# Attention on one Trainium2 core: the value products cut in three parts, one in each slot of the loop

## The chip, the core and the metric

The kernel runs on one core of one Trainium2 chip. TensorE (PE) multiplies, VectorE (DVE) and ScalarE (ACT) empty PSUM and do the element work, GpSimd (POOL) prepares operands and issues some DMAs, SyncE (SP) issues the rest. PSUM has eight banks of 128 x 512 fp32. The metric is the device time of one execution in microseconds (us).

## The reference, cut to what matters

The program is an attention block (16 heads of 768 x 64, scores masked by a hash of queries and keys), then a Fourier mixing layer with an MLP, then a second mixing layer. The change touches the attention alone:

```
q_bits = (einsum('bhsd,dk->bhsk', q, proj) > 0);  k_bits likewise
mask   = q_bucket[:, :, :, None] == k_bucket[:, :, None, :]
scores = where(mask, q @ k.T / sqrt(64), -1e9)
attn   = exp(scores - max);  attn /= sum(attn) + 1e-9
out    = attn @ v
```

## The kernel before, in words

**Slots.** Each head has six tiles of 128 query rows against 768 keys. schedule() makes a list of slots, one for each tile n = 6h + t, and every engine walks that list in order. "Slot t of head h" below is the slot of tile n. In it stand, for each engine:

- PE: four score products of tile n (L765, L766, into one of two pairs of banks), six transposes of the exponentials of tile n - 2 (L740, two ring banks named eta and etb), then value products if the slot has any (L779, L780), then its units: "bits" (three hash products of a half of the next head's queries and keys, L718 to L720 with 24 columns) or "back" (three transposes of a finished half of the output, L751).
- DVE: the row maximum (L984) and the affine pair of tile n (L987), the low halves ETL of tile n - 2 (L994), and for a back unit the inverse sums and the addition OS (L1014 to L1020).
- ACT: the high halves ETH of tile n - 2 (L613), the exponential of tile n (L633), copies for units (MB L622, OL L627), and OS, the copy of finished value products out of PSUM (L642).

fp32 data are split in a high part that the multiplier takes whole and the rest: ETH and ETL, TOPH and TOPL, VHL (both parts of v side by side).

**Value products.** A head has two of them, (h, 0) and (h, 1), one for each half of its query rows: 12 matmuls of 384 columns into one ring bank. Before the change (h, 0) stands whole in slot 5 of head h, and (h, 1) whole in slot 2 of head h + 1. The last matmul raises s_pv.

**The ring.** The eta, etb, bits, back and value products take the four banks 4 to 7 in turn; take_bank() waits until the engine that empties the bank four units ago has done so.

**GpSimd's queue.** It runs in program order, once per head: split_top(h + 1), which writes TOPH and TOPL of the next head (L498, L500); mask_rows, MR (L505); finish(h - 1, 0), which scales an output half into X (L513); split_v(h + 1), VHL (L529, L531), which waits until s_pv shows that all value products of head h - 1 are done, since it overwrites their VHL; scale_q(h + 2) on QK (L490); finish(h - 1, 1). In the first eight heads a table or weight DMA is issued twice a head (L556). The bits products of a head wait for its TOPH and TOPL (s_top), and its score products for the mask rows and for DMAs that SP issues once TOPL and the bits are there.

Of the kernel before, what the change touches and what calls it, by code (L numbers as in the profile page):

```python
# [7 lines left out]
ACT = mybir.ActivationFunctionType  # L8
# [5 lines left out]
NH = B * H  # L14
# [20 lines left out]
FOLD = [NH * QT + 2 + i for i in range(3)]  # L35
LAG = 2
NE = LAG + 1
RING = 4
NSTAT = 4 * QT
TG = 5  # L40
WIDTHS = (P, P, 1, P, P - 1)
# [8 lines left out]
def schedule():  # L50


    slots = [(None, None, None, [("bits", 0, i) for i in range(2)])]
    for n in range(NH * QT + 5):
        h, t = divmod(n, QT)
        pv = (h - 1, 1) if t == 2 and h else (h, 0) if t == 5 and h < NH else None
        units = []
        if h + 1 < NH and t == 1:
            units += [("bits", h + 1, i) for i in range(2)]
        if h and t in (1, 4):  # L60
            units.append(("back", h - 1, t // 4))
        slots.append((n if n < NH * QT else None, n - LAG if LAG <= n < NH * QT + LAG else None, pv, units))
    return slots


def program(nc, qk, v, projb, w1, w2, wth, wtr, wti, wch, ident_in, gamma_in, sign_in, cs_in, ss_in, alt_in, cd_in, sd_in, out):
# [126 lines left out]
    with ctx:  # L193
# [11 lines left out]
            return PS[:, 4 + u % RING, :]  # L205


        def blocks(ap):
            return ap.rearrange("p (a b) -> p a b", b=P)

# [2 lines left out]
        for _, et, pv, us in slots:  # L213
            if et is not None:
                units += [("eta", *divmod(et, QT)), ("etb", *divmod(et, QT))]
            if pv is not None:
                units.append(("pv", *pv))
            units += us
        unit_no = {u: i for i, u in enumerate(units)}
        done = {}  # L220
        for u in units:
            done[u] = len([w for w in done if w[0] != "pv"]) + 1
        nth, seen = {}, {}
        for u in units:
            seen[u[0]] = nth[u] = seen.get(u[0], 0) + 1
# [247 lines left out]
        def _(pool):  # L473
# [18 lines left out]
            def split_top(h):  # L492
                b = h % 2
                pool.wait_ge(s_sq, h)
                pool.wait_ge(s_top, 2 * h)
                if h >= 2:
                    pool.wait_ge(s_s, QT * (h - 1))
                nc.gpsimd.tensor_copy(TOPH[:, b], QK[:, b]).then_inc(s_top, 1)  # L498
                pool.wait_ge(s_top, 2 * h + 1)
                nc.gpsimd.tensor_tensor(TOPL[:, b], QK[:, b], TOPH[:, b].bitcast(F32), ALU.subtract).then_inc(s_top, 1)  # L500

            def mask_rows(h):
                pool.wait_ge(emptied["bits"], 2 * (h + 1))
                pool.wait_ge(s_mask, 32 * h)
                nc.gpsimd.tensor_scalar(MR[:], MB[:], gamma[:, 0:1], gamma[:, 1:2], ALU.is_gt, ALU.mult).then_inc(s_mr, 1)  # L505
# [29 lines left out]
            scale_q(1)  # L535
            for slot, (tile, et, pv, us) in enumerate(slots):
                h, t = divmod(slot - 1, QT)
                if slot and t == 0 and h + 1 < NH:
                    split_top(h + 1)
                if slot and t == 1:  # L540
                    if h + 1 < NH:
                        mask_rows(h + 1)
                    if h:
                        finish(h - 1, 0)
                if slot and t == 2:
                    if h == 0:
                        split_v(0)
                    if h + 1 < NH:
                        split_v(h + 1)
                    if h + 2 < NH:  # L550
                        scale_q(h + 2)
                if slot and t == 4 and h:
                    finish(h - 1, 1)
                if slot and t in (3, 5) and early:
                    dst, src, landed = early.pop(0)
                    pool.dma_start(dst, src).then_inc(landed, 16)  # L556
            pool.wait_ge(s_pv, 2 * NH)
            split_low(n_w1)
            for n in range(NT):
# [27 lines left out]
        def _(act):  # L587
# [16 lines left out]
            for slot, (tile, et, pv, us) in enumerate(slots):  # L604
                if et is not None:
                    h, t = divmod(et, QT)
                    for k, kind in enumerate(("eta", "etb")):
                        u = unit_no[kind, h, t]
                        bank = blocks(ring(u)[:, 0:HC])
                        act.wait_ge(s_ring, done[kind, h, t])  # L610
                        if h and k == 0:
                            act.wait_ge(s_pv, 2 * h + t // HALF - 1)
                        nc.scalar.activation(ETH[:, t // HALF, k * HALF:(k + 1) * HALF, (t % HALF) * P:(t % HALF + 1) * P],  # L613
                                             bank, ACT.Copy).then_inc(s_eth, 1)
                for u in us:
                    kind, h, i = u
                    c = slice(i * HC, (i + 1) * HC)
                    if kind == "bits" and h:
                        act.wait_ge(s_ring, done[u])
                        if h >= 2:  # L620
                            act.wait_ge(s_mr, h - 1)
                        nc.scalar.activation(MB[:, c], ring(unit_no[u])[0:2 * NM, 0:HC], ACT.Copy).then_inc(emptied["bits"], 1)  # L622
                    elif kind == "back":
                        act.wait_ge(s_ring, done[u])
                        if h:
                            act.wait_ge(emptied["back"], nth[u] - 2)
                        nc.scalar.activation(OL2[:, i], blocks(ring(unit_no[u])[:, 0:HC])[:, :, D:P], ACT.Copy).then_inc(s_ol, 1)  # L627
                if tile is not None:
                    t = tile % NSTAT
                    act.wait_ge(s_sb, tile + 1)  # L630
                    if tile >= NE:
                        act.wait_ge(s_ring, done["etb", (tile - NE) // QT, (tile - NE) % QT])
                    nc.scalar.activation(E[:, tile % NE, :], s_bank(tile)[:, 0:S], ACT.Exp, bias=affine[:, t, 1:2],  # L633
                                         scale=affine[:, t, 0:1], accum_out=esum[:, t:t + 1]).then_inc(s_exp, 1)
                if slot in FOLD[1:]:
                    fold_high(0, FOLD.index(slot) - 1)
                if pv is not None:
                    h, c = pv
                    act.wait_ge(s_pv, 2 * h + c + 1)
                    if h >= 1:  # L640
                        act.wait_ge(s_ring, done["back", h - 1, c])
                    nc.scalar.activation(OS[:, c, :], ring(unit_no["pv", h, c])[:, 0:HC], ACT.Copy).then_inc(emptied["pv"], 1)  # L642

            for b in range(B):
                for g in range(TG):
# [69 lines left out]
        def _(pe):  # L715
# [38 lines left out]
            for tile, et, pv, us in slots:  # L754
                if tile is not None:
                    h, t = divmod(tile, QT)
                    pe.wait_ge(s_away, 32 * (h + 1))
                    pe.wait_ge(s_in, 32 * (h + 1))
                    pe.wait_ge(s_mask, 32 * (h + 1))
                    if tile >= 2:  # L760
                        pe.wait_ge(s_exp, tile - 1)
                    c = slice(t * P, (t + 1) * P)
                    for lo, hi in ((0, 512), (512, S)):
                        dst = s_bank(tile)[:, lo:hi]
                        nc.tensor.matmul(dst, TOPL[:, h % 2, c], TOPH[:, h % 2, lo:hi], start=True, stop=False)  # L765
                        last = nc.tensor.matmul(dst, QM[:, h % 2, c], KM[:, h % 2, lo:hi], start=False, stop=True)  # L766
                    last.then_inc(s_s, 1)
                if et is not None:
                    unit(("eta", *divmod(et, QT)))
                    unit(("etb", *divmod(et, QT)))  # L770
                if pv is not None:
                    h, c = pv
                    pe.wait_ge(s_vs, 2 * h + 2)
                    pe.wait_ge(emptied["eta"], h * QT + (c + 1) * HALF)
                    pe.wait_ge(emptied["etb"], h * QT + (c + 1) * HALF)
                    take_bank(unit_no["pv", h, c])
                    bank = ring(unit_no["pv", h, c])
                    for j in range(QT):
                        nc.tensor.matmul(bank[:, 0:HC], VHL[:, h % 2, j, :], ETH[:, c, j, :], start=(j == 0), stop=False)  # L779
                        last = nc.tensor.matmul(bank[:, 0:HC], VHL[:, h % 2, j, :], ETL[:, c, j, :], start=False, stop=(j == QT - 1))  # L780
                    last.then_inc(s_pv, 1)
                for u in us:
                    unit(u)

# [11 lines left out]
            for b in range(B):  # L796
# [18 lines left out]
                if b:  # L815
                    norm_transpose(0)
                    norm_transpose(1)
                else:
                    pe.wait_ge(emptied["back"], seen["back"])

                def cosines(dst, cols):
                    for g in range(2):
# [414 lines left out]
```

## Time and profile before

| | us |
|---|---|
| median of 3 runs | 825.1 (821.96 to 827.07) |
| the profiled execution | 824.21, span 821.4 |
| attention, first score product to last ETL | 14.2 to 279.3 of the span |
| PE busy / DVE / ACT / POOL in the span | 753.2 / 451.6 / 313.2 / 269.5 |

The times in the rows are from the start of the span. A row of the timeline gives the start, the duration, engine, line, operation, output and inputs, shapes, and the number of instructions merged in it; in brackets stands how long the engine had been idle before it and what ended that. A matmul's duration holds its way through the array, so the pitch, from one start to the next, is what it occupies.

### The profile page before, as it was taken

The numbers are of one execution on the slowest core, as the hardware profiler recorded it, in microseconds if no ns is written. First come the engines' busy times: TensorE is split into PE (matmuls) and PEld (weight loads), VectorE is DVE, ScalarE is ACT, GpSimd is POOL, SyncE is SP. The second block draws the span as 40 slices with busy tenths as digits, with TensorE's granted clock in tenths as the row PEclk, the third lists the DMA queues.
The fourth block names the chain that finished last, engine by engine and source line by source line (L and its number), as shares of the span: only waits on it lengthen the run. The fifth ranks groups of instructions, "written<-read, shape, count | busy, mean of one in ns | idle before, by whom it ended". The sixth has DMA issues, their size and how long they took to land.

```text
span 821.4 us, 11002 instructions
## 1 busy us (share of the span) xinstructions
PE 753.2 (92%) x3826; PEld 624.3 (76%) x3826; DVE 451.6 (55%) x834; ACT 313.2 (38%) x659; POOL 269.5 (33%) x243
## 2 busy tenths in 40 slices
PE   4899899999999679699999999999996898999998
PEld 2778787878788556588888888888884787888876
DVE  2888889888888967722222111211117665756433
ACT  2787877788778602210110111111113433222201
POOL 3867677656662167453200000110001214221100
PEclk9999999999999966889999999999999999999999
DMA  5354546543321023631100000400003222000002
GB/s 147 96 144 114 149 110 186 173 105 98 84 72 43 1 102 129 204 103 40 39 1 0 1 1 0 129 14 1 0 1 90 78 58 71 1 14 13 26 26 77
DMA packets 44680, 56.26 MB, mean 68 GB/s; under 512 B 15956, under 2 KB 27860, under 8 KB 44116
## 3 DMA queue, kind: packets, MB, share of 16 engines
q1 hardware_dynamic: 38100, 41.65, 18.3%
q0 software_dynamic: 6528, 13.92, 5.8%
q8 instruction: 32, 0.52, 0.3%
q14 instruction: 20, 0.16, 0.1%
HBM read 38.65 MB, written 3.15 MB: 51 GB/s over the span
## 4 chain that ended last, share of the span: by engine, by line
PE 75%; DVE 19%; issue 3%; DMA 1%; ACT 1%; SPq 1%; POOL 0%; ACTq 0%; POOLq 0%
PE PS L718 19%; PE PS L720 18%; PE PS L719 18%; DVE negmax L984 6%; DVE ETL L994 5%; PE PS L779 4%; PE PS L780 3%; PE PS L765 3%; DVE affine L987 3%; PE PS L740 3%; PE PS L766 3%; PE PS L898 1%; PE PS L751 1%; PE PS L905 1%; PE PS L790 1%
## 5 line engine op out<-in xcount | busy, mean ns | idle before, releaser
L1109 DVE SCALAR_TENSOR_TENSOR HL<-PS,HH 128x512 fp32r<-128x512 f32 x48 | 33.2, 692 | 189.2 <-ACT HH L681 189.2
L633 ACT ACTIVATE E<-PS,affine 128x768 f32<-128x768 f32 x96 | 95.6, 995 | 42.0 <-DVE affine L987 42.0
L984 DVE TENSOR_REDUCE negmax<-PS 128x1 f32<-128x768 f32 x96 | 91.2, 951 | 34.8 <-PE PS L766 34.7
L681 ACT ACTIVATE HH<-PS 128x512 fp32r<-128x512 f32 x48 | 28.7, 598 | 210.5 <-PE PS L720 210.5
L994 DVE TENSOR_TENSOR ETL<-PS,ETH 128x384 fp32r<-128x384 f32 x192 | 97.1, 547 | 1.0 <-ACT ETH L613 1.0
L613 ACT ACTIVATE ETH<-PS 128x384 fp32r<-128x384 f32 x192 | 83.2, 489 | 10.8 <-PE PS L740 10.5
L740 PE MATMUL PS<-ident,E 128*128 128x128 f32 x576 | 81.7, 274 | 0.0
L765 PE MATMUL PS<-TOPH,TOPL 128*128 128x512 f32 x192 | 71.4, 372 | 10.3 <-DMA KM<-MR 6.0
L718 PE MATMUL PS<-UTH,W1H 128*128 128x512 f32 x192 | 76.7, 400 | 2.1 <-DVE UTL L1092 2.1
L720 PE MATMUL PS<-UTH,W1L 128*128 128x512 f32 x192 | 75.8, 395 | 0.0
L719 PE MATMUL PS<-UTL,W1H 128*128 128x512 f32 x192 | 75.7, 394 | 0.0
L720 PE MATMUL PS<-W2H,HL 128*128 128x512 f32 x192 | 74.7, 389 | 0.0
L718 PE MATMUL PS<-W2H,HH 128*128 128x512 f32 x192 | 74.7, 389 | 0.0
L719 PE MATMUL PS<-W2L,HH 128*128 128x512 f32 x192 | 74.7, 389 | 0.0
L779 PE MATMUL PS<-ETH,VHL 128*128 128x384 f32 x192 | 67.3, 350 | 3.5 <-DVE ETL L994 1.7
L740 PEld LDWEIGHTS PS<-ident,E 128*128 128x128 f32 x576 | 65.6, 141 | 3.4 <-DVE ETL L994 3.4
L581 POOL TENSOR_TENSOR ZF<-X,SC 128x512 f32<-128x512 f32 x24 | 30.5, 1291 | 106.9 <-ACT SC L702 106.9
L780 PE MATMUL PS<-ETL,VHL 128*128 128x384 f32 x192 | 64.8, 338 | 0.0
L766 PE MATMUL PS<-KM,QM 76*128 76x512 f32 x192 | 62.6, 346 | 0.0
L505 POOL TENSOR_SCALAR MR<-MB,gamma 24x768 fp32r<-24x768 f32 x15 | 44.1, 2942 | 51.0 <-ACT MB L622 51.0
L718 PE MATMUL PS<-ZH,WTH 128*128 128x512 f32 x144 | 59.8, 415 | 0.0
L720 PE MATMUL PS<-ZH,WTL 128*128 128x512 f32 x144 | 57.0, 396 | 0.0
(167 smaller groups left out, 1516.8 us busy)
## 6 DMA issues: line engine op xcount, KB each, us to landing
stage<-in_moe_w_ch_dram SPq DMA_DIRECT2D x36, 256.0 KB, 2.6
QK<-in_qk_dram SPq DMA_DIRECT2D x16, 384.0 KB, 3.8
W1H<-in_moe_w_ch_dram POOLq DMA_DIRECT2D x4, 1024.0 KB, 5.7
W2H<-in_moe_w_ch_dram POOLq DMA_DIRECT2D x4, 1024.0 KB, 8.8
QM<-TOPH SPq DMA_DIRECT2D x16, 192.0 KB, 2.8
KM<-TOPL SPq DMA_DIRECT2D x16, 192.0 KB, 3.1
TOPL<-QM SPq DMA_DIRECT2D x16, 192.0 KB, 2.7
TOPH<-TOPH SPq DMA_DIRECT2D x16, 192.0 KB, 3.0
```

The lines of the kernel that those rows point to most:

```text
L613: nc.scalar.activation(ETH[:, t // HALF, k * HALF:(k + 1) * HALF, (t % HALF) * P:(t % HALF + 1) * P], bank, ACT.Copy).then_inc(s_eth, 1)
L633: nc.scalar.activation(E[:, tile % NE, :], s_bank(tile)[:, 0:S], ACT.Exp, bias=affine[:, t, 1:2], scale=affine[:, t, 0:1], accum_out=esum[ ...
L718: nc.tensor.matmul(dst, hl, hr, start=start, stop=False)
L719: nc.tensor.matmul(dst, hl, lr, start=False, stop=False)
L720: return nc.tensor.matmul(dst, ll, hr, start=False, stop=stop)
L740: last = nc.tensor.transpose(bank[:, j * P:(j + 1) * P], E[:, tile % NE, (first + j) * P:(first + j + 1) * P], ident[:])
L765: nc.tensor.matmul(dst, TOPL[:, h % 2, c], TOPH[:, h % 2, lo:hi], start=True, stop=False)
L766: last = nc.tensor.matmul(dst, QM[:, h % 2, c], KM[:, h % 2, lo:hi], start=False, stop=True)
L779: nc.tensor.matmul(bank[:, 0:HC], VHL[:, h % 2, j, :], ETH[:, c, j, :], start=(j == 0), stop=False)
L780: last = nc.tensor.matmul(bank[:, 0:HC], VHL[:, h % 2, j, :], ETL[:, c, j, :], start=False, stop=(j == QT - 1))
L984: nc.vector.tensor_reduce(negmax[:, t, 1:2], s_bank(tile)[:, 0:S], AX_X, ALU.max, negate=True).then_inc(s_max, 1)
L994: nc.vector.tensor_tensor(ETL[where], blocks(ring(unit_no[kind, h, t])[:, 0:HC]), ETH[where].bitcast(F32), ALU.subtract).then_inc(emptied[ ...
```

## The change

The value products of a half are cut in three parts of four matmuls. With PVLAG = 5 the part of tile p = n - 5 stands in slot n, so every slot from the fifth on has one: parts 2 and 3 of (h - 1, 0) in slots 0 and 1 of head h, those of (h - 1, 1) in slots 2, 3 and 4, and part 1 of (h, 0) in slot 5. All of them accumulate in a bank of their own, OT (bank 7), and the first part of a half waits until ACT has copied the half before out of it. The ring has three banks, without the value products. Units are one a slot at most: bits in slots 0 and 1 (both were in slot 1), back in slots 3 and 5 (they were in 1 and 4). On ACT the exponential now stands ahead of the copies OS, MB and OL. On GpSimd, split_top(h + 2) stands in slot 5 of head h where split_top(h + 1) stood in slot 0, and the finish calls come later.

```diff
-RING = 4
+RING = 3
+PVLAG = 5
...
-    for n in range(NH * QT + 5):
+    for n in range(NH * QT + QT):
         h, t = divmod(n, QT)
-        pv = (h - 1, 1) if t == 2 and h else (h, 0) if t == 5 and h < NH else None
         units = []
-        if h + 1 < NH and t == 1:
-            units += [("bits", h + 1, i) for i in range(2)]
-        if h and t in (1, 4):
-            units.append(("back", h - 1, t // 4))
+        if h + 1 < NH and t < 2:
+            units.append(("bits", h + 1, t))
+        if h and t in (3, 5):
+            units.append(("back", h - 1, t // 5))
+        p = n - PVLAG
+        pv = (p // QT, p % QT // HALF, p % HALF) if 0 <= p < NH * QT else None
...
+        OT = PS[:, 7, 0:HC]
...
-                if slot and t == 0 and h + 1 < NH:
-                    split_top(h + 1)
-                if slot and t == 1:
-                    if h + 1 < NH:
-                        mask_rows(h + 1)
-                    if h:
-                        finish(h - 1, 0)
+                if slot and t == 0:
+                    if h == 0:
+                        split_top(1)
+                    elif h > 1:
+                        finish(h - 2, 1)
+                if slot and t == 1 and h + 1 < NH:
+                    mask_rows(h + 1)
                 if slot and t == 2:
...
                         split_v(h + 1)
                     if h + 2 < NH:
                         scale_q(h + 2)
-                if slot and t == 4 and h:
-                    finish(h - 1, 1)
-                if slot and t in (3, 5) and early:
+                if slot and t == 3 and h:
+                    finish(h - 1, 0)
+                if slot and t == 5 and h + 2 < NH:
+                    split_top(h + 2)
+                if slot and t in (2, 4) and early:
...
+            finish(NH - 1, 1)
...
-                if pv is not None:
-                    h, c = pv
-                    act.wait_ge(s_pv, 2 * h + c + 1)
-                    if h >= 1:
-                        act.wait_ge(s_ring, done["back", h - 1, c])
-                    nc.scalar.activation(OS[:, c, :], ring(unit_no["pv", h, c])[:, 0:HC], ACT.Copy).then_inc(emptied["pv"], 1)
+                if pv is not None and pv[2] == HALF - 1:
+                    h, c, _ = pv
+                    act.wait_ge(s_pv, 2 * h + c + 1)
+                    if h:
+                        act.wait_ge(s_ring, done["back", h - 1, c])
+                    nc.scalar.activation(OS[:, c, :], OT, ACT.Copy).then_inc(emptied["pv"], 1)
...
-                    h, c = pv
-                    pe.wait_ge(s_vs, 2 * h + 2)
-                    pe.wait_ge(emptied["eta"], h * QT + (c + 1) * HALF)
-                    pe.wait_ge(emptied["etb"], h * QT + (c + 1) * HALF)
-                    take_bank(unit_no["pv", h, c])
-                    bank = ring(unit_no["pv", h, c])
-                    for j in range(QT):
+                    h, c, part = pv
+                    if part == 0:
+                        pe.wait_ge(s_vs, 2 * h + 2)
+                        pe.wait_ge(emptied["eta"], h * QT + (c + 1) * HALF)
+                        pe.wait_ge(emptied["etb"], h * QT + (c + 1) * HALF)
+                        if h or c:
+                            pe.wait_ge(emptied["pv"], 2 * h + c)
+                    for j in range(2 * part, 2 * part + 2):
...
-                    last.then_inc(s_pv, 1)
+                    if part == HALF - 1:
+                        last.then_inc(s_pv, 1)
```

GpSimd's queue before, with the semaphores that each instruction waits for (s_pv: value products done; s_sum: back additions done; s_qk0: queries and keys loaded). The piece begins in slot 1 of a head, at the mask rows:

```order
L505 TENSOR_SCALAR MR<-MB,gamma 24x768 [waits s_mask,s_bits]
L513 TENSOR_TENSOR X<-OS_68,einv 128x3x64 [waits s_sum,s_inv]
L529 CAST VHL<-VR 128x6x64 [waits s_pv,s_v1]
L531 TENSOR_TENSOR VHL<-VR,VHL 128x6x64 [waits s_vs]
L490 TENSOR_SCALAR QK<-QK 64x768 [waits s_qk0]
L556 DMA W1H<-in_moe_w_ch_dram 128x2048
L513 TENSOR_TENSOR X<-OS_68,einv 128x3x64 [waits s_sum,s_inv]
L556 DMA W1H<-in_moe_w_ch_dram 128x2048
L498 CAST TOPH<-QK 128x768 [waits s_s,s_top,s_sq]
L500 TENSOR_TENSOR TOPL<-QK,TOPH 128x768 [waits s_top]
```

The same stretch now, from the mask rows of the same head (line numbers shift by two to six):

```order
L507 TENSOR_SCALAR MR<-MB,gamma 24x768 [waits s_mask,s_bits]
L531 CAST VHL<-VR 128x6x64 [waits s_pv,s_v1]
L533 TENSOR_TENSOR VHL<-VR,VHL 128x6x64 [waits s_vs]
L492 TENSOR_SCALAR QK<-QK 64x768 [waits s_qk0]
L560 DMA W1H<-in_moe_w_ch_dram 128x2048
L515 TENSOR_TENSOR X<-OS_68,einv 128x3x64 [waits s_sum,s_inv]
L560 DMA W1H<-in_moe_w_ch_dram 128x2048
L500 CAST TOPH<-QK 128x768 [waits s_s,s_top,s_sq]
L502 TENSOR_TENSOR TOPL<-QK,TOPH 128x768 [waits s_top]
L515 TENSOR_TENSOR X<-OS_68,einv 128x3x64 [waits s_sum,s_inv]
```

From VHL to TOPL the instructions are the same but for their finish: one X stood before VHL and one between the DMAs; now one stands between the DMAs and one behind TOPL.

PE now, from the end of slot 5 of one head to the first bits product in slot 0 of the next; the value products of slot 5 wait for s_os, the copy of the half before out of OT, and the bits product for s_top:

```order
L785 MATMUL PS<-ETH,VHL 128x384 [waits s_etb,s_os,s_eta,s_vs]
L786 MATMUL PS<-ETL,VHL 128x384
L785 MATMUL PS<-ETH,VHL 128x384
L786 MATMUL PS<-ETL,VHL 128x384
L756 MATMUL PS<-ident,OS 128x128 [waits s_os,s_etb]
L756 MATMUL PS<-ident,OS 128x128 x2
L770 MATMUL PS<-TOPH,TOPL 128x512 [waits s_mask,s_exp,s_in,s_away]
...
L785 MATMUL PS<-ETH,VHL 128x384
L786 MATMUL PS<-ETL,VHL 128x384
L723 MATMUL PS<-TOPH,projH 24x384 [waits s_top,s_sum]
```

Before, slot 5 had twelve value products in one row and slot 0 none, and the bits stood one slot later, behind the transposes of slot 1.

## Rows read from the trace of the kernel before

**Rows 1.** Busy time in a stretch: us, PE, PEld, DVE, ACT, POOL, clock, DMA
```profile
140.00:180.00 40.00, 36.86 (x229) 31.46 (x228) 35.62 (x75) 31.18 (x72) 25.99 (x23) 1.00 0.46 132
```

**Rows 2.** Timeline of PE, slots 1 to 4 of head 7
```profile
134.59 0.55 PE L751 MATMUL PS<-ident,OS 128*128 128x128 f32 x3 [0.61 <-DVE ETL L994]
134.89 0.48 PE L765 MATMUL PS<-TOPH,TOPL 128*128 128x512 f32 x1
...
136.25 0.42 PE L779 MATMUL PS<-ETH,VHL 128*128 128x384 f32 x1
136.51 0.34 PE L780 MATMUL PS<-ETL,VHL 128*128 128x384 f32 x1
...
138.43 0.39 PE L765 MATMUL PS<-TOPH,TOPL 128*128 128x512 f32 x1
...
139.13 0.82 PE L740 MATMUL PS<-ident,E 128*128 128x128 f32 x6
139.71 0.48 PE L765 MATMUL PS<-TOPH,TOPL 128*128 128x512 f32 x1
```

**Rows 3.** Timeline of DVE, the same head
```profile
132.92 0.95 DVE L984 TENSOR_REDUCE negmax<-PS 128x1 f32<-128x768 f32 x1
134.91 0.16 DVE L1014 TENSOR_SCALAR einv<-esum 128x3 f32<-128x3 f32 x1
135.88 0.96 DVE L984 TENSOR_REDUCE negmax<-PS 128x1 f32<-128x768 f32 x1
140.32 0.81 DVE L987 SCALAR_TENSOR_TENSOR affine<-negmax 128x2 f32<-128x2 f32 x1
```

**Rows 4.** Timeline of POOL, the same head
```profile
138.73 0.50 POOL L529 CAST VHL<-VR 128x384 fp32r<-128x384 f32 x1 [0.45 <-PE PS L780]
140.29 2.13 POOL L490 TENSOR_SCALAR QK<-QK 64x768 f32<-64x768 f32 x1
144.75 0.50 POOL L513 TENSOR_TENSOR X<-OS,einv 128x192 f32<-128x192 f32 x1 [1.75 <-DVE OS L1020]
145.21 0.60 POOL L556 DMA_DIRECT2D W1H<-in_moe_w_ch_dram  x1
145.81 0.84 POOL L498 CAST TOPH<-QK 128x768 fp32r<-128x768 f32 x1
146.74 1.83 POOL L500 TENSOR_TENSOR TOPL<-QK,TOPH 128x768 fp32r<-128x768 f32 x1
```

**Rows 5.** Timeline of ACT, the same head
```profile
137.11 1.01 ACT L633 ACTIVATE E<-PS,affine 128x768 f32<-128x768 f32 x1
138.63 0.49 ACT L642 ACTIVATE OS<-PS 128x384 f32<-128x384 f32 x1 [0.42 <-PE PS L780]
```

**Rows 6.** The DMAs on POOL, by tile: ns min/median/max; two of ten rows
```profile
L556 POOL DMA_DIRECT2D W1H<-in_moe_w_ch_dram x4: 594/604/618, 125.8 to 145.2; - x4
L556 POOL DMA_DIRECT2D CSH<-in_cs_dram x1: 874/874/874, 42.2 to 42.2; - x1
```

**Rows 7.** Timeline: first bits products of heads 2 and 15, TOPL of head 2, last ETL
```profile
29.95 1.83 POOL L500 TENSOR_TENSOR TOPL<-QK,TOPH 128x768 fp32r<-128x768 f32 x1
32.51 0.42 PE L718 MATMUL PS<-TOPH,projH 128*24 128x384 f32 x1
...
248.23 0.42 PE L718 MATMUL PS<-TOPH,projH 128*24 128x384 f32 x1
...
277.38 1.95 DVE L994 TENSOR_TENSOR ETL<-PS,ETH 128x384 fp32r<-128x384 f32 x4 [1.01 <-ACT ETH L613]
```

**Rows 8.** Timeline of PE, behind gaps; then a stretch of PE: busy, granted clock, DMA, GB/s
```profile
345.10 0.45 PE L790 MATMUL PS<-ident,UN 128*128 128x128 f32 x1 [3.29 <-DVE UTL L1092]
...
634.99 0.52 PE L905 MATMUL PS<-ident,nat 128*128 128x128 f32 x3 [1.73 <-DVE TR L1141]
...
688.57 0.52 PE L905 MATMUL PS<-ident,nat 128*128 128x128 f32 x3 [2.21 <-DVE WTL L1131]
...
344.50:354.60 10.10, 7.38 (x21) 0.50 0.46 131
689.30:692.50 3.20, 3.20 (x11) 0.50 0.09 31
```

More of the change, by code:

```diff
@@ L215, in program @@
                 units += [("eta", *divmod(et, QT)), ("etb", *divmod(et, QT))]
-            if pv is not None:
-                units.append(("pv", *pv))
             units += us
@@ L221, in program @@
         for u in units:
-            done[u] = len([w for w in done if w[0] != "pv"]) + 1
+            done[u] = len(done) + 1
         nth, seen = {}, {}
@@ L614, in _ @@
                                              bank, ACT.Copy).then_inc(s_eth, 1)
+                if tile is not None:
+                    t = tile % NSTAT
+                    act.wait_ge(s_sb, tile + 1)
+                    if tile >= NE:
+                        act.wait_ge(s_ring, done["etb", (tile - NE) // QT, (tile - NE) % QT])
+                    nc.scalar.activation(E[:, tile % NE, :], s_bank(tile)[:, 0:S], ACT.Exp, bias=affine[:, t, 1:2],
+                                         scale=affine[:, t, 0:1], accum_out=esum[:, t:t + 1]).then_inc(s_exp, 1)
+                if slot in FOLD[1:]:
+                    fold_high(0, FOLD.index(slot) - 1)
+                if pv is not None and pv[2] == HALF - 1:
[4 more added lines that the diff above has]
+                    nc.scalar.activation(OS[:, c, :], OT, ACT.Copy).then_inc(emptied["pv"], 1)
                 for u in us:
@@ L627, in _ @@
                         nc.scalar.activation(OL2[:, i], blocks(ring(unit_no[u])[:, 0:HC])[:, :, D:P], ACT.Copy).then_inc(s_ol, 1)
[L628 to L637, printed above, removed]
-                    h, c = pv
-                    act.wait_ge(s_pv, 2 * h + c + 1)
-                    if h >= 1:
-                        act.wait_ge(s_ring, done["back", h - 1, c])
-                    nc.scalar.activation(OS[:, c, :], ring(unit_no["pv", h, c])[:, 0:HC], ACT.Copy).then_inc(emptied["pv"], 1)
             for b in range(B):
@@ L771, in _ @@
                 if pv is not None:
-                    h, c = pv
-                    pe.wait_ge(s_vs, 2 * h + 2)
-                    pe.wait_ge(emptied["eta"], h * QT + (c + 1) * HALF)
-                    pe.wait_ge(emptied["etb"], h * QT + (c + 1) * HALF)
-                    take_bank(unit_no["pv", h, c])
-                    bank = ring(unit_no["pv", h, c])
-                    for j in range(QT):
-                        nc.tensor.matmul(bank[:, 0:HC], VHL[:, h % 2, j, :], ETH[:, c, j, :], start=(j == 0), stop=False)
-                        last = nc.tensor.matmul(bank[:, 0:HC], VHL[:, h % 2, j, :], ETL[:, c, j, :], start=False, stop=(j == QT - 1))
-                    last.then_inc(s_pv, 1)
+                    h, c, part = pv
[6 more added lines that the diff above has]
+                    for j in range(2 * part, 2 * part + 2):
+                        nc.tensor.matmul(OT, VHL[:, h % 2, j, :], ETH[:, c, j, :], start=(j == 0), stop=False)
+                        last = nc.tensor.matmul(OT, VHL[:, h % 2, j, :], ETL[:, c, j, :], start=False, stop=(j == QT - 1))
+                    if part == HALF - 1:
+                        last.then_inc(s_pv, 1)
                 for u in us:
@@ L819, in _ @@
                     pe.wait_ge(emptied["back"], seen["back"])
+                    pe.wait_ge(emptied["pv"], 2 * NH)
                 def cosines(dst, cols):
```

## The prediction, made before the changed kernel ran

> **What bounds it now.** I read three views: busy time by stretch, then the timelines of one head, engine by engine, then PE's idle times and its clock. In the middle of the attention PE is busy 36.9 of 40 us, DVE 35.6, ACT 31.2, at full clock [rows 1]. So no engine is alone the bound. The unit is the head: from the first bits product of head 2 (in head 1) to that of head 15 (in head 14) lie 248.23 - 32.51 = 215.7 us for 13 heads, 16.6 a head [rows 7].
>
> What must PE do in a head? From the pitches: score products 138.43 to 139.13, 0.70; six transposes 139.13 to 139.71, 0.58; twelve value products 136.25 to 138.43, 2.18, that is 0.26 for the first behind transposes and 0.175 for each other; a back unit 0.30 [rows 2], and the score product behind it is 0.08 dearer, as one behind transposes is. Bits matmuls have the same 384 columns: three are 0.52. What must DVE do? A slot without back is 132.92 to 134.91, 2.0; the back work 134.91 to 135.88 adds 1.0 [rows 3]. Before, PE has a slot of S + T + 2.18 = 3.5 us where DVE has only 2.0 to do, and slots where DVE needs longer than PE: neither can be busy all the time. That is what an even spread of the value products removes.
>
> **The change, first by engine loads alone.** PE's slots become 0.70 + 0.58 + 0.26 + 3 x 0.175 = 2.05 bare, 2.57 with bits, 2.43 with back: 2 x 2.57 + 2 x 2.05 + 2 x 2.43 = 14.1 a head. DVE's: 6 x 2.0 + 2 x 1.0 = 14.0, and about 1.1 more of affine instructions held up while GpSimd works: one is 0.81 long [rows 3], where the others are 0.16, and two or so a head are. So by loads a head could take 15.1 instead of 16.6.
>
> Does DVE's hold-up stay? The row shows an affine held 0.65 beside the QK scaling, which runs 2.13 [rows 3, 4]. The Trainium skill (SBUF — State Buffer, two separate sides) says that a VectorE instruction with two SBUF inputs and a GpSimd instruction exclude each other for the whole instruction; by that the row would be over 2 long, and the head 15.1 + 1.3 = 16.4, most of the gain gone. Here the affine came free 0.8 after the scaling began, so the row speaks for a part of it only, and I keep 1.1.
>
> **Then by waits: GpSimd's queue.** split_v(h + 1) stands in front of scale_q(h + 2), finish(h - 1, 0) and split_top(h + 2), and waits for the last value product of head h - 1. That stood in slot 2 of head h; VHL was written 0.30 after its end (138.43 to 138.73), having waited 0.45 [rows 2, 4]. Now its last part is in slot 4: two slots later. And the one who waits for split_top(h + 2), the bits product, has gone from slot 1 of the next head to slot 0, one slot earlier. Before, TOPL of head 2 was there at 31.78 and its bits came at 32.51 [rows 7]: 0.7 of slack in the whole head. The change takes about three slots from it. I follow the loop:
>
> - GpSimd, from the end of the value products in slot 4: 0.30 to VHL; VHL and the QK scaling, 138.73 to 142.42, 3.69; one finish 0.46 (144.75 to 145.21); TOPH and TOPL 145.81 to 148.57, 2.76; the signal to PE about 0.1. Sum 7.3 [rows 4].
> - PE, from that same point to where the bits are due: slot 5, 2.43, slot 0, 2.05, so 4.5; and 0.4 of wait for OT (below). PE stands idle 7.3 - 4.9 = 2.4 us at the bits.
> - PE, from the bits to the next end of slot 4: 0.52 + 2.57 + 2.05 + 2.43 + 2.05 = 9.6. DVE in slots 1 to 4 has 9.0, begins 1.2 behind the bits, and needs its backs at 3.0, so it keeps up with PE. The period is 9.6 + 7.3 = 16.9.
> - In heads 1 to 7 two DMAs stand in the chain, 0.59 to 0.87 each, a little under 0.04 of it beside other work [rows 6]: 14 of them, 9.3 in all, 1.3 a head, period 18.2. Before, they lay in GpSimd's slack.
>
> So 13 periods: 13 x 16.9 + 9.3 = 229.0 against 215.7: **+13.3**.
>
> The ends. Bits of head 1 now stand between the first two score tiles, at low clock (0.96); the mask rows and all behind them on GpSimd come about 1.15 later, and TOPL of head 2 at 32.9 instead of 31.78: **+0.5**. After the bits of head 15 nothing waits for GpSimd. Before, 248.23 to the end of the last ETL, 279.33, took 31.1 [rows 7]. Now: to the first score tile of head 15, 0.52 + 2.57 + 2.05 + 2.43 + 2.05 + 2.43 and 0.4 for OT, 12.4; five slots, by DVE 11.0; the last tile to its ETL 5.6 (score 0.7, DVE's queue 3.0 and twice 0.95). Sum 29.0: **-2.1**. Behind that the fold of the first batch sets the pace as before, and the last back now comes behind more ACT work; I cost it at 0, from -0.5 to +1.
>
> Costed at nothing, and by what: the ring of three. The second transposes of a slot need the bank that DVE empties a slot earlier, due 0.5 to 1.0 us before. ACT has 1.8 for ETH and E a slot and is not full [rows 1, 5]. The mask rows reach their DMAs about 8 us after the bits, and score products need them 12 after. If one of these covers fails it costs 0.3 to 0.8 a head.
>
> The wait for OT, for which no row exists: lower bound 0 (PE comes later than the copy), upper bound E and OS behind a late maximum. In slot 4 DVE starts its maximum 0.5 late, because the back add of slot 3 is before it; then 1.15 to the affine's end, E 1.0, OS 0.5 [rows 3, 5] makes it 0.4 later than PE arrives in slot 5. It falls in the shadow of the GpSimd chain, so its 0.4 only shortens the idle time above.
>
> Sum on the profiled execution's 824.2: 13.3 + 0.5 - 2.1 = +11.7, 835.9, if the clock stays.
>
> **The clock.** PE is now idle 2.4 us once a head, 3.7 with the DMAs. Gaps of 2.21 and 3.29 were followed by stretches at a granted clock of 0.50, that is 1.2 GHz, of 3 and 10 us; one of 1.73 was not [rows 8]. At half the clock a slot with bits grows by about 0.44 (bits) + 0.70 (score) + 0.55 (value) = 1.7, on 2.57; over some 3.4 us that is 1.3 to 1.6 lost, and it lies in the 9.6 of the loop, so it counts in full. I take it for 5 of the 7 long gaps and 3 of the 6 short ones (2.4 lies near the row of 2.21, and one row is no rule), 8 x 1.4, less a quarter that falls into the gap itself: **+8**. Bounds: 0, and 13 x 1.6 = 21. The Trainium skill (TensorE: Matmul & The Clock Gate, on oscillation) warns against idle gaps, and by its rule the short gaps are harmless and the DMA heads at the edge; that would give +0 to +9, and the row of 2.21 speaks against its harmless part.
>
> **Forecast:** 824.2 + 11.7 + 8 = 844; the profiled execution is 0.9 below the median of the runs, which is inside the rounding; I say 844. Attention ends near 299 instead of 279.
>
> **Rivals.**
> - *The chain is there, the clock holds*: 836 to 838. For it: the gap of 1.73, after which it held [rows 8]; against it, the other two. Chance 0.20; the forecast with some falls (839 to 849) 0.48.
> - *Falls in nearly every head*, by the 2.21 row: 824.2 + 11.7 + 16 to 21 = 852 to 857. Chance 0.14.
> - *Faster: the chain does not bind.* If TOPL is ready when PE comes to the bits, loads decide: 15.1 a head, 1.5 less for 14 heads, 824 - 21 = **804**. It decides at a chain under 4.9 us from the end of slot 4; the rows give 7.3. It would need s_pv to be satisfied earlier than the order of the queues says. Chance 0.05.
> - *Little change*: the loop is there, but the tail and the clock behind the attention fall well (the three runs differ by 5 us), and PE's slots are shorter than I add: 826 to 833. Chance 0.10. The remaining 0.03 is a loss from a cover gone (ring, mask DMAs): up to 865.
>
> About 1% is what one can tell here. Faster by over 1% (under 817): 0.05. Within: 0.10. Slower: 0.85. The range, 831 to 857, leaves out the fast case, most of the small change and the top.
>
> **What would show it.** GpSimd's VHL cast ended by PE's value product once a head, with an idle time of several us; PE's first bits product (24 columns) in slot 0 idle 2 to 4 us, ended by GpSimd's TOPL; heads 18 to 20 us apart up to head 7 and 17 to 18 after it; less busy DVE and PE in each head. DVE waiting for PE once a head. Heads 14 and 15 shorter than before. Wrong if the bits do not wait for TOPL, if the period is under 16.5, or if the clock falls and the period is unmoved by it.

## The result, and the profile after

The changed kernel takes 847.3 us (median of 4 runs, 844.1 to 856.6) against 824.3; the ratio is 1.030, 95% interval 1.021 to 1.038. Forecast were 844 and a range of 831 to 857. The profiled execution took 848.04, its span 845.3 instead of 821.4.

Where do the 23.9 us of the spans lie? The last ETL ends at 306.86; before, at 279.33 [rows 7]. So the attention is 27.5 longer, and all that follows 3.6 shorter, in which nothing was changed: its low-clock stretches fall differently from execution to execution, 44 us of them before and 38 now. I therefore compare attention ends from here on, and give the times beside them.

First the page of the changed kernel: busy time, then the chain that ended last.

```profile
PE 752.8 (89%) x3826; PEld 629.7 (74%) x3826; DVE 455.6 (54%) x834; ACT 318.4 (38%) x659; POOL 268.0 (32%) x243
...
PE 75%; POOL 12%; DVE 5%; issue 3%; ACT 2%; DMA 1%; SPq 1%; POOLq 0%; ACTq 0%
```

The same work as before, to 2%. But the chain goes through POOL for 12% of the span where it had 0%, and through DVE for 5% instead of 19%. Which waits are new? From the list of waits: engine, line and who ended them; us in total, times, longest.

```profile
POOL VHL L531 <- PE PS L786: 38.9, 14, 3.3
...
PE PS L723 <- POOL TOPL L502: 35.5, 14, 3.6
```

These two are the loop: GpSimd waits 14 times for the last value product (the VHL cast), then TensorE 14 times for TOPL. One turn of it, POOL's timeline in heads 11 and 12, which have no DMAs:

```profile
223.31 1.80 POOL L502 TENSOR_TENSOR TOPL<-QK,TOPH 128x768 fp32r<-128x768 f32 x1
225.07 0.51 POOL L515 TENSOR_TENSOR X<-OS,einv 128x192 f32<-128x192 f32 x1
229.80 2.93 POOL L507 TENSOR_SCALAR MR<-MB,gamma 24x768 fp32r<-24x768 f32 x1 [4.22 <-ACT MB L642]
235.21 0.50 POOL L531 CAST VHL<-VR 128x384 fp32r<-128x384 f32 x1 [2.48 <-PE PS L786]
235.79 1.01 POOL L533 TENSOR_TENSOR VHL<-VR,VHL 128x384 fp32r<-128x384 f32 x1
236.78 2.13 POOL L492 TENSOR_SCALAR QK<-QK 64x768 f32<-64x768 f32 x1
238.89 0.50 POOL L515 TENSOR_TENSOR X<-OS,einv 128x192 f32<-128x192 f32 x1
239.34 0.82 POOL L500 CAST TOPH<-QK 128x768 fp32r<-128x768 f32 x1
240.24 1.81 POOL L502 TENSOR_TENSOR TOPL<-QK,TOPH 128x768 fp32r<-128x768 f32 x1
```

and PE's first bits products in the same two heads:

```profile
225.26 0.33 PE L723 MATMUL PS<-TOPH,projH 128*24 128x384 f32 x1 [1.49 <-POOL TOPL L502]
...
242.19 0.34 PE L723 MATMUL PS<-TOPH,projH 128*24 128x384 f32 x1 [1.48 <-POOL TOPL L502]
```

Compare with [rows 4]: the VHL cast waited 0.45 there and 2.48 here. From it to the bits, 235.21 to 242.19, 6.98; with the 0.30 ahead of it the 7.3 of the forecast. From the bits at 225.26 to the end of slot 4 (0.30 before the cast, 234.91) 9.65, forecast 9.6. The period is 16.93 in each of six heads; the seven ahead of them, in which DMAs are issued, take 18.2 to 21.5. Two of these begin like this (PE's timeline):

```profile
33.60 0.49 PE L723 MATMUL PS<-TOPH,projH 128*24 128x384 f32 x1 [3.65 <-POOL TOPL L502]
...
55.05 0.49 PE L723 MATMUL PS<-TOPH,projH 128*24 128x384 f32 x1 [3.62 <-POOL TOPL L502]
```

The stretches behind them, by windows: the stretch and its length, busy us (instructions) of PE, of its weight loads, DVE, ACT and POOL, then the granted clock, DMA share and GB/s.

```profile
34.00:39.00 5.00, 5.00 (x19) 4.18 (x18) 2.23 (x4) 2.65 (x6) 0.00 (x0) 0.50 0.58 161
56.00:60.00 4.00, 4.00 (x16) 3.62 (x15) 2.23 (x4) 2.20 (x4) 0.00 (x0) 0.50 0.77 215
```

0.50 is the lower of the two levels, 1.2 GHz. PE is busy for the whole of these 5 and 4 us, as it would be for half as long at full clock. Six of the eight long gaps were followed by such a stretch (gaps of 3.65, 3.62, 3.35, 3.40, 3.54 and 2.73; not those of 3.17 and 3.14), none of the six gaps of 1.5. In three of the six the clock was down before the gap ended.

### The profile page after: what moved, and what is told of

Read it like the earlier page. It is cut to its first block, busy times and chain, and to the rows that moved or that the text cites. A ratio compares the mean times of both kernels' runs of the same rounds, so it can differ in the third digit from the quotient of the medians.

```text
span 845.3 us, 11003 instructions
## 1 busy us (share of the span) xinstructions
PE 752.8 (89%) x3826; PEld 629.7 (74%) x3826; DVE 455.6 (54%) x834; ACT 318.4 (38%) x659; POOL 268.0 (32%) x243
## 4 chain that ended last, share of the span: by engine, by line
PE 75%; POOL 12%; DVE 5%; issue 3%; ACT 2%; DMA 1%; SPq 1%; POOLq 0%; ACTq 0%
PE PS L723 19%; PE PS L725 18%; PE PS L724 18%; PE PS L745 5%; POOL QK L492 4%; POOL TOPL L502 3%; PE PS L770 3%; PE PS L785 3%; PE PS L771 3%; PE PS L786 3%; POOL TOPH L500 1%; PE PS L906 1%; POOL VHL L531 1%; PE PS L913 1%; POOL VHL L533 1%
## 5 line engine op out<-in xcount | busy, mean ns | idle before, releaser
L745 PE MATMUL PS<-ident,E 128*128 128x128 f32 x576 | 84.5, 282 | 1.2
L785 PE MATMUL PS<-ETH,VHL 128*128 128x384 f32 x192 | 75.1, 391 | 8.9 <-ACT OS L634 6.3
L745 PEld LDWEIGHTS PS<-ident,E 128*128 128x128 f32 x576 | 68.2, 145 | 3.8 <-DVE ETL L1002 3.5
L786 PE MATMUL PS<-ETL,VHL 128*128 128x384 f32 x192 | 66.9, 348 | 0.0
```

The lines of the kernel that those rows point to most:

```text
L745: last = nc.tensor.transpose(bank[:, j * P:(j + 1) * P], E[:, tile % NE, (first + j) * P:(first + j + 1) * P], ident[:])
L785: nc.tensor.matmul(OT, VHL[:, h % 2, j, :], ETH[:, c, j, :], start=(j == 0), stop=False)
L786: last = nc.tensor.matmul(OT, VHL[:, h % 2, j, :], ETL[:, c, j, :], start=False, stop=(j == QT - 1))
```

## The experiments

Theory A: GpSimd's queue closes a loop, and PE's idle gap in it lowers the clock. Theory B: the smaller ring and the single bank OT cost the time. All were timed beside the kernel before, whose median was 823.9 with the first four and 824.5 with the others. Attention ends are those of the profiled executions.

**v behind TOP.** In GpSimd's queue of the changed kernel:

```diff
                     if h == 0:
                         split_v(0)
-                    if h + 1 < NH:
-                        split_v(h + 1)
+                        split_v(1)
...
-                if slot and t == 5 and h + 2 < NH:
-                    split_top(h + 2)
+                if slot and t == 5:
+                    if h + 2 < NH:
+                        split_top(h + 2)
+                    if 0 < h < NH - 1:
+                        split_v(h + 1)
```

Expected: 

> The changed kernel with one call of GpSimd moved: the split of v for the next head (VHL) stands behind the split of TOPH and TOPL in slot 5, no longer ahead of it in slot 2, so that nothing the bits products wait for stands behind the wait for the value products. Theory A (GpSimd's queue is the loop that sets the head, and its idle gap makes the clock fall): the gap at the bits goes, the period is set by the loads, 15.1 us a head, attention ends near 258, the time is 804 (800 to 812). Theory B (the ring of three and the single bank OT cost the time): the gap moves to other waits, the period stays above 16.5, the time stays over 835.

Measured: 814.3 (ten runs, 811.7 to 817.3), ratio to before 0.988 (0.984 to 0.991); attention end 272.9, 34 earlier than in the changed kernel. All gaps at the bits but the first are gone. One call's place in one queue turns a loss of 3% into a gain of 1.2%. Ring, OT and value products are as in the changed kernel, so B falls as the main cause. But 804 was missed: heads 3 to 6 take 15.1 to 15.5, as expected, but head 2 takes 15.6, head 7, the last with DMAs, 16.25, and those without DMAs 16.0; and the first gap stayed, with 6.8 us of low clock behind it. The 16.0 are taken up under "v ahead in late heads".

**DMAs in slot 1.** The two DMAs a head issued behind mask_rows instead of in slots 2 and 4:

```diff
                 if slot and t == 1 and h + 1 < NH:
                     mask_rows(h + 1)
+                    for _ in range(2 if h else 0):
+                        if early:
+                            dst, src, landed = early.pop(0)
+                            pool.dma_start(dst, src).then_inc(landed, 16)
...
-                if slot and t in (2, 4) and early:
-                    dst, src, landed = early.pop(0)
-                    pool.dma_start(dst, src).then_inc(landed, 16)
```

Expected: 

> The changed kernel with the two DMAs a head that GpSimd issues in slots 2 and 4 issued in slot 1, behind the mask rows, where GpSimd is idle 2.5 to 3.1 us. Theory A: GpSimd's chain loses 1.3 us in seven heads, every gap is 1.5 as in heads 8 to 13, the clock does not fall in the attention, all periods are 16.93; 7 x (20.12 - 16.93) = 22 less: 825 (822 to 829). If the falls have nothing to do with the gap's length, they stay: 9 less, 838.

Measured: 831.8 (829.0 to 835.9), 15 less than the changed kernel; attention end 287.2, 19.7 less. Heads 2 to 6 take 16.93 to 16.96, as the late heads do: the DMAs' 1.3 and the falls that came with them are gone. The clock fell twice even so, after gaps of 2.00 and 1.96, and not after gaps of 1.95 and 2.04. Heads 7 to 9 take 17.6 to 18.2. In 7 and 8 another wait came up, on PE, and 9 begins at low clock:

```profile
150.51 0.47 PE L771 MATMUL PS<-TOPH,TOPL 128*128 128x512 f32 x1 [2.04 <-DMA KM<-MR]
```

Two 1 MB weight DMAs are now issued from 142.53 on, and the mask rows' small one, which the score product waits for, at 143.43; it let PE go 7.1 us later. That the large loads hold it up is likely, but not shown. Of the 7 us by which 825 was missed, 2.6 lie in the attention of the profiled execution (1.6 lost in head 1, behind the first fall, and 2.7 in heads 7 to 9, less 1.8 gained ahead of the bits of head 2), 1.3 behind it, and the rest between executions.

**Before, with ring of three.** The kernel before, with value products whole and in their old slots, but in bank 7:

```diff
-RING = 4
+RING = 3
...
+        OT = PS[:, 7, 0:HC]
...
-            if pv is not None:
-                units.append(("pv", *pv))
...
-                    take_bank(unit_no["pv", h, c])
-                    bank = ring(unit_no["pv", h, c])
+                    if h or c:
+                        pe.wait_ge(emptied["pv"], 2 * h + c)
+                    bank = PS[:, 7, :]
...
```

Expected: 

> The kernel before with one part of the change: the value products whole and in their old slots, but in a bank of their own (bank 7), with the wait for its copy, and the ring of three banks. Theory A: no GpSimd wait is changed; the three-bank ring costs a few tenths a head at the slot with bits and back together: 826 to 832. Theory B (the ring and OT are the loss): 840 to 850.

Measured: 826.9 (825.3 to 832.0), ratio 1.005 (1.001 to 1.008); attention end 285.6, 6.3 later than before, most heads 17.1 instead of 16.5. PE's timeline shows a wait at the bits, where the kernel before has none there and one of 0.61 at the back transposes behind them [rows 2]:

```profile
187.44 0.36 PE L718 MATMUL PS<-TOPH,projH 128*24 128x384 f32 x1 [0.83 <-DVE ETL L996]
```

So B has a true part, 0.6 a head, in this order of slots, where bits and back stand together; how much of it is the ring and how much OT, the run does not tell. In the changed order it does not come on top: its late periods are the 7.3 and the 9.65 of the loop, and the first experiment, with the same ring and OT, has heads of 15.1 to 15.5.

**Filler in the gap.** In front of the first bits product of eight heads:

```diff
+                    if 2 <= h <= 9 and i == 0:
+                        for _ in range(14):
+                            nc.tensor.matmul(bank[:, 0:HC], TOPH[:, (h - 1) % 2, 0:P], TOPH[:, (h - 1) % 2, 0:HC], start=True, stop=True)
```

Expected: 

> The changed kernel with 14 matmuls of 384 columns (2.5 us, into the bits' own bank, overwritten by the bits) in front of the first bits product in the eight heads whose gap is 2.7 to 3.7 us. They add no work to the chain, since PE is idle there. Theory A with the clock as its second term: the clock does not fall, these periods go from 20.1 to the 18.2 that the one head without a fall has: 7 x 1.9 + 1.5 = 15 less, 832 (829 to 836). If the long periods come from longer waits on GpSimd and not from the clock: 847 as the changed kernel, or a little more.

Measured: 841.6 (836.0 to 845.0); attention end 294.1, 12.7 earlier than the changed kernel, though PE does 112 matmuls more. PE's timeline, one filler and the bits behind it:

```profile
85.76 2.62 PE L751 MATMUL PS<-TOPH 128*128 128x384 f32 x14
88.81 0.36 PE L723 MATMUL PS<-TOPH,projH 128*24 128x384 f32 x1 [0.44 <-POOL TOPL L502]
```

and by windows one of the stretches shown above:

```profile
34.00:39.00 5.00, 5.00 (x35) 4.57 (x34) 3.52 (x7) 3.94 (x9) 0.97 (x1) 1.00 0.74 193
```

35 matmuls in those 5 us instead of 19. PE still waits for TOPL, but the clock holds in the whole attention, and the seven periods with DMAs are 18.1 to 18.6, 18.3 in the mean, instead of 20.1. That is the price of the clock: 12.7. The time fell by only 6, 4 between the two profiled executions, and there the part behind the attention explains it: it took 548 in this execution, 58 us of it at low clock (27 on end), and 538 in the changed kernel's, 38 of it at low clock.

**v ahead in late heads.** To the first experiment's slot 5:

```diff
                 if slot and t == 5:
+                    if 8 <= h < NH - 1:
+                        split_v(h + 1)
                     if h + 2 < NH:
                         split_top(h + 2)
-                    if 0 < h < NH - 1:
+                    if 0 < h < 8:
                         split_v(h + 1)
```

Expected: 

> The kernel of the run v_behind_top, with the split of v ahead of the split of TOPH and TOPL in slot 5 from head 8 on. In that run the heads with DMAs on GpSimd take 15.3 to 15.4 us and those without 16.0, though GpSimd has less to do there: there an affine instruction of VectorE falls on the 1.83 us TOPL split and takes 1.3, and the inverse sums behind it 0.7. Theory (VectorE and GpSimd exclude each other, and the phase of the two decides): TOPL comes 1.5 later, the affine takes 0.16 to 0.2, heads 8 to 13 fall to 15.3 to 15.5, 4 us less than that run: 810. Rival (the heads differ by something else, such as the DMAs in flight): heads 8 to 13 stay at 16.0, the time at 814.

Measured: 810.6 (four runs, 809.3 to 814.2), ratio 0.983 (0.979 to 0.988); attention end 267.8, 5.1 earlier. Heads 8 to 13 take 15.3 to 15.4 each. What was it that cost 0.7 a head? The timeline of the first experiment, head 11, POOL and DVE:

```profile
205.69 1.83 POOL L502 TENSOR_TENSOR TOPL<-QK,TOPH 128x768 fp32r<-128x768 f32 x1
...
206.25 1.29 DVE L997 SCALAR_TENSOR_TENSOR affine<-negmax 128x2 f32<-128x2 f32 x1
```

An affine instruction of 0.16 lasted to the end of TOPL, and E waited for it. In this run, in the same head:

```profile
203.30 0.16 DVE L999 SCALAR_TENSOR_TENSOR affine<-negmax 128x2 f32<-128x2 f32 x1
203.39 1.84 POOL L502 TENSOR_TENSOR TOPL<-QK,TOPH 128x768 fp32r<-128x768 f32 x1
204.32 0.94 DVE L1026 TENSOR_SCALAR einv<-esum 128x3 f32<-128x3 f32 x1
```

The affine is through before TOPL, and what falls on it is the inverse sums (0.94 instead of 0.16), which ended with it. The rival, the table and weight DMAs in flight, is out: GpSimd issues none in those heads in either run.

**First head.** In addition split_v(1) behind split_top(2), no DMAs in head 0, and the other order from head 9 on:

```diff
                         split_v(0)
-                        split_v(1)
...
-                    if 8 <= h < NH - 1:
+                    if 9 <= h < NH - 1:
...
-                    if 0 < h < 8:
+                    if h < 9:
                         split_v(h + 1)
-                if slot and t in (2, 4) and early:
+                if slot and h and t in (2, 4) and early:
```

Expected: 

> The kernel above, and in head 0 only one split of v ahead of the split for head 2 and no DMAs; all 16 DMAs one head later, the other order from head 9 on. The gap of 3.7 us at the bits of head 2, with the fall of the clock behind it, shrinks to under 1.5: 3.7 - 2.8 - and 2 to 3 of low clock: 4 to 5 less than the run above: 806. If PE's wait there is on something else than GpSimd (the DMA of QK), the gap stays and so does the time.

Measured: 810.7 (four runs, 800.0 to 812.9), ratio, of the three fastest, 0.977 (0.969 to 0.985); attention end 261.8, 5.9 earlier. The gap at the bits of head 2 is down to 0.17, and its low clock is gone, as expected; but behind the attention the profiled execution took 546 instead of 540. The median did not move, and the runs are too few and too wide to say more.

**OS first.** In addition, ScalarE copies OT ahead of the exponential; the block is moved up in its slot:

```diff
+                if pv is not None and pv[2] == HALF - 1:
+                    h, c, _ = pv
+                    act.wait_ge(s_pv, 2 * h + c + 1)
...
+                    nc.scalar.activation(OS[:, c, :], OT, ACT.Copy).then_inc(emptied["pv"], 1)
                 if tile is not None:
```

Expected: 

> The kernel above, and on ScalarE the copy OS out of the bank OT stands ahead of the exponential in its slot. Theory: of a head, 2 x 0.6 us are PE's wait for OT, which comes because the copy stands behind E, itself behind the affine; with the copy first the waits go, and up to 0.6 a head comes back where PE is the bound, nothing where VectorE is (14.4 of 15.4 us busy): 800 to 806. Rival: the exponential comes 0.7 later twice a head and VectorE's next maximum waits for it: 806 to 812.

Measured: 806.5 (six runs, 802.4 to 807.5), ratio 0.977 (0.973 to 0.981); attention end 263.8, 2.0 later than without. PE's wait for the copy is gone, and a late head takes 15.5 instead of 15.34: the rival was right in the sign. VectorE's affine instructions now meet GpSimd for longer (0.285 in the mean of late heads against 0.249); with six a head that is 0.2, as much as was lost, but that it is the cause is not shown. The lower time lies behind the attention, in the profiled executions 540 in one and 546 in the other. By their times these two are not told apart.

**Bits a slot later.** The changed kernel with one edit:

```diff
-        if h + 1 < NH and t < 2:
-            units.append(("bits", h + 1, t))
+        if h + 1 < NH and t in (1, 2):
+            units.append(("bits", h + 1, t - 1))
```

Expected: 

> The changed kernel with the bits products in slots 1 and 2 instead of 0 and 1, and nothing else: GpSimd's queue and the value products stay as the change has them. It gives the chain from the value products to the bits 2.1 to 2.6 us more. Theory A: the gap of 1.5 in heads 8 to 13 goes, that of 2.7 to 3.7 shrinks to about 1, the clock holds: periods 15.4 to 16.2, then the mask rows' DMAs may be late for the score products by 0.2 to 0.6: 814 to 822. Theory B (not the chain, but the small slots): 840 or more.

Measured: 821.6 (ten runs), ratio 0.997 (0.993 to 1.000); attention end 278.0, 29 earlier than the changed kernel. The loop is met from its other end, and one slot of room is enough to break even. The heads with DMAs take 16.1 to 16.6, with gaps of 1.1 to 1.6 at the bits. But the late heads take 16.55, not 15.4 to 16.2, and the wait is not on the mask rows as I had thought. PE waits for VectorE's ETL, which frees a bank of the ring; the rows of GpSimd, VectorE and PE there:

```profile
196.33 1.81 POOL L502 TENSOR_TENSOR TOPL<-QK,TOPH 128x768 fp32r<-128x768 f32 x1
196.40 1.76 DVE L995 SCALAR_TENSOR_TENSOR affine<-negmax 128x2 f32<-128x2 f32 x1
198.08 1.01 DVE L1002 TENSOR_TENSOR ETL<-PS,ETH 128x384 fp32r<-128x384 f32 x2
198.68 0.55 PE L745 MATMUL PS<-ident,E 128*128 128x128 f32 x3 [1.26 <-DVE ETL L1002]
```

So this wait is in the first place what the run above of late heads showed: an affine, 0.16 alone, begins just behind TOPL and lasts to TOPL's end, and ETL comes 1.6 late for it. The ring of three hands that on to PE; what a fourth bank would give back is not shown.

## Why the prediction was right, point by point

| attention, us | forecast | measured |
|---|---|---|
| to the bits of head 2 | +0.5 | +1.1 (33.60 against 32.51; 0.5 of it is a later start) |
| 13 periods without the clock | +13.3 | +14.1 (7 x 18.32 with filler, 6 x 16.93, less 215.7) |
| the clock in them | +8 | +12.6 |
| from the bits of head 15 to the last ETL | -2.1 | -0.3 (30.8 against 31.1) |
| sum | +20 | +27.5 |
| behind the attention | 0 | -3.6 |

- **The loop** was right in place and size: 7.3 and 9.6, period 16.9. The engine loads alone, and the busy shares, would have forecast a gain.
- **The idle gap** was too long in the forecast: 2.4 and 3.7, measured 1.5 and 2.7 to 3.7. PE loses more on its way to the bits: from the end of slot 4 to its last value product 5.6 instead of 4.9. That is the wait for OT: the six transposes of slot 5 begin at 235.62 and take 0.58 alone, and the value products behind them begin at 237.37, 1.2 later than these would let them, where the forecast had 0.4. The period does not depend on it, since GpSimd's side of the loop is the longer.
- **The clock** was the term sized worst. Six falls in the eight long gaps was near the mark; each cost about 2, not 1.4 less a quarter. Three of them lasted 6.8 us and three 3.4, and of these 31 us at low clock only 4 lay in the gaps. Against that, three of the short gaps were counted that did not fall. Two errors in part cancelled.
- **The time** came nearer than its parts: the attention was forecast 7.5 too short, and 3.6 of it came back behind the attention, where nothing was changed. That is luck; the range would have held without it.
- **Which gaps bring the clock down?** Six of 1.5 did not; one of 1.96 in the second experiment did, and one of 3.17 did not, so length alone does not say it. The Trainium skill (TensorE: Matmul & The Clock Gate, on oscillation) has a rule by which short gaps are harmless; the six gaps of 1.5 agree with it, the one of 1.96 does not.
- **VectorE's hold-up.** The affine that falls on TOPL lasts to TOPL's end at 225.11. Beside the scaling of QK it is as in the forecast: an affine begun with the scaling comes free after 0.8 of 2.1. But the inverse sums, begun 1.8 behind the scaling's start at 236.78, take 0.36 instead of 0.16 and end with it:

```profile
223.54 1.60 DVE L995 SCALAR_TENSOR_TENSOR affine<-negmax 128x2 f32<-128x2 f32 x1
...
238.58 0.36 DVE L1022 TENSOR_SCALAR einv<-esum 128x3 f32<-128x3 f32 x1
```

The Trainium skill's rule (SBUF — State Buffer, two separate sides), that the two engines exclude each other for the whole instruction, agrees with the row of TOPL; with the affine beside the scaling it does not.
- **The last heads** gained 0.3, not 2.1. From the bits of head 15 to its first score tile (289.19) it took 13.1, forecast 12.4; the five slots to 300.32 took 11.1, forecast 11.0; the last tile took 6.5, forecast 5.6. In the first and the third of these PE waited for OT, and its value products began 1.2 and 0.7 late.
- **The rival "faster"** had its price right in kind: with the chain out of the way the time was 814 and, with GpSimd's order improved further, 806 to 811, not 804.

## What to carry to other kernels

When work is spread over a loop's slots to balance engines, follow every wait that used to hang on its end: here a buffer was freed two slots later, and the one in-order queue behind that wait carried, four instructions on, what another engine needed a slot earlier. Put the wait that is not urgent last in the queue. And price an idle gap of TensorE at more than its length: here six of the eight gaps of 2.7 to 3.7 us each cost about 2 us more by the clock.

## What the runs showed of the hardware that I had not expected

VectorE's inverse sums, one input of three elements, are held by GpSimd's two-input split as the affine is: 0.94 instead of 0.16. GpSimd's one-input scaling of QK, 2.13 long, holds VectorE's affine for about its first 0.8 us, and inverse sums begun 1.7 to 1.8 into it until its end; why these two differ no run here shows. And more work can be faster: 112 useless matmuls in idle gaps brought the attention's end 12.7 us forward. The same unchanged 540 us behind the attention took from 538 to 548 in these profiles, with 34 to 58 us of it at low clock (38 at 538, 58 at 548).
